# One change to a fused attention, mixer and routed-expert kernel: nine of twelve token tiles routed inside the last mixer block

## The chip, the cores and the metric

The kernel runs on one core of a Trainium2 chip. Its time is the device time of one execution in microseconds (us). Each engine of the core (TensorE, VectorE, ScalarE, GpSimd, SyncE) works through its own queue in order; semaphores tie the queues together. In rows, PE is TensorE's matmuls, PEld its weight loads, DVE is VectorE, ACT ScalarE, POOL GpSimd and SP SyncE.

## The reference

Three layers follow each other, all in fp32:

```python
def reference(...):
    attn_out = _attn_ref(q, k, v, n_global, n_local)      # (2, 8, 768, 64), windowed attention with bias
    x = attn_out.transpose(0, 2, 1, 3).reshape(B, S, H * D)   # (2, 768, 512)
    # mixer
    u = x + ((x.transpose(0, 2, 1) @ U) @ V).transpose(0, 2, 1)     # rank 32 over the sequence
    x = u + np.maximum(u @ w_ch1, 0) @ w_ch2                  # 512 -> 2048 -> 512
    # routed experts: E = 8, F = 1024
    logits = x @ w_gate;  local_gate = sigmoid(x @ w_local)
    for b in range(B):
        for s in range(S):
            fresh_e = argmax(logits[b, s])
            e = fresh_e if s == 0 or local_gate[b, s] < 0.5 else prev_e
            prev_e = e
            p = softmax(logits[b, s])
            out[b, s] = p[e] * (np.maximum(x[b, s] @ w1[e], 0) @ w2[e])
```

A token's expert depends on the token before it, where the local gate says so. The 1536 tokens are twelve token tiles of 128.

## The kernel before, in words

Every weight and activation is kept as a high and a low part (fp32r), and each product is three matmuls (`passes`, L477), so weights are cast on ScalarE (`split_hi`, L629) and their remainder made on VectorE (`split_lo`, L633), in eight units of 128 x 1024 for each of two weight buffers. `wbuf[0]` holds the mixer's first matrix, `wbuf[1]` its second; the experts then use the two by turns.

The mixer works in four blocks (kb) of three token tiles. A block has sixteen steps (f): `up` of f into a PSUM bank, `relu` on ScalarE (L714), its low part on VectorE (L751), and, one step behind, `down` of f-1 into three banks. At the end of a block VectorE adds the banks to `x` (`add_block`, L735), SyncE stores the three tiles to DRAM (`store_mixed`, L1205), and in steps 2 to 5 of the next block TensorE turns them and makes their gate logits (L544, L558), nine columns wide.

After the last block come the last three tiles' turning (L613) and logits (L620), and then, once logits of all twelve tiles are there, the routing: `route_dve` is a chain of small linked VectorE operations, each of which waits for the one before, and `route_pe_part` gives it TensorE's answers (turned rows L878, chain ends L882, carry L886, chain back L888, counts L891 to L893, places L898). The last of these is a 0/1 matmul that yields, for every expert tile, which token rows it takes and with which gate. GpSimd then gathers the 128 rows of the first expert tile from DRAM (`gather`, L1107, L1109), TensorE turns them (L932) and the loop over experts 0 to 7 begins. Each expert has one tile for every 128 of its tokens; while its first tile runs, the next expert's eight units are split. A tile is 24 `up` matmuls, 24 `down` matmuls and three groups of four transposes; its result is scaled (L1056) and scattered to the output (L1122) during the next tile.

TensorE's order around the change: all mixer steps, tail turns, tail logits, routing matmuls, first turn, tiles. ScalarE and VectorE split the first expert's units only after the mixer's last `up`, VectorE partly between routing operations. SyncE loads expert 0's first four units in the middle of the mixer, the other four in block 3.

## Time and profile before

| | |
|---|---|
| median of 3 runs | 631.56 us (631.07 to 634.59) |
| profiled execution, its own time | 633.74 us |
| its span, first to last instruction | 632.1 us |
| mean granted TensorE clock | 0.964 |
| TensorE busy | 590.1 us (93%), 3238 matmul instructions |
| VectorE / ScalarE / GpSimd busy | 267.6 / 242.9 / 125.5 us |
| last mixer block | 324.5 to 397.8 us of the span |
| first expert tile starts | 432.7 us |

An fp32 matmul shows as two instructions in a row's count, an fp32r one as one. Durations of neighbouring matmuls overlap, so the time from start to start is what a sequence takes. "[idle before <-releaser]" at the end of a row is how long the engine had sat idle and what ended it.

### The profile page before, as it was taken

To read this page: it belongs to the slowest core of one execution; us is meant where nothing else is said; L and a number is where in the kernel's file an instruction comes from. 1 tells how busy PE (TensorE), PEld (TensorE's weight loads), DVE (VectorE), ACT (ScalarE), POOL (GpSimd) and SP (SyncE) were. 2 spreads that over 40 slices of the span, in tenths; PEclk is the share of its full clock that TensorE was granted. 3 is DMA by queue.
4 is the path that set the end of the run, shared out by engine and by line. 5 is a ranking of instruction groups with operands and counts; after the bars stand their busy time and mean duration, and the time that the engine had idled before them with its cause. 6 is when DMAs were issued, how large, how long until landed. Compare 5 with 4: busy or idle time off the path is not lost.

```text
span 632.1 us, 9619 instructions
## 1 busy us (share of the span) xinstructions
PE 590.1 (93%) x3238; PEld 519.1 (82%) x3239; DVE 267.6 (42%) x566; ACT 242.9 (38%) x423; POOL 125.5 (20%) x160
## 2 busy tenths in 40 slices
PE   4999999999999999999999999646999999999995
PEld 4999898998899899999889999444787887888884
DVE  6565475444321221212221111785846278557311
ACT  6988584333112111111112011505734276537121
POOL 2999980000000000000000000002312122122121
PEclk9999997999999999999999999756999999999998
DMA  8678522433110000100000300535948169471110
GB/s 323 234 268 312 228 90 68 160 133 101 66 51 1 0 1 2 50 1 1 0 36 16 102 32 1 183 104 178 345 155 290 50 212 335 136 258 39 40 46 24
DMA packets 25252, 73.79 MB, mean 117 GB/s; under 512 B 2895, under 2 KB 4447, under 8 KB 25216
## 3 DMA queue, kind: packets, MB, share of 16 engines
q1 hardware_dynamic: 22128, 65.37, 29.1%
q0 software_dynamic: 2672, 7.62, 3.5%
q8 instruction: 21, 0.34, 0.2%
q10 hardware_dynamic: 416, 0.33, 0.2%
q14 instruction: 15, 0.12, 0.1%
HBM read 67.02 MB, written 7.34 MB: 118 GB/s over the span
## 4 chain that ended last, share of the span: by engine, by line
PE 76%; POOL 7%; DVE 6%; issue 5%; DMA 2%; ACT 2%; ACTq 1%; SPq 1%; DVEq 0%; POOLq 0%
PE bank L477 62%; POOL k_parts L1535 3%; DVE wbuf L633 3%; POOL q_parts L1532 2%; PE bank L959 2%; PE bank L521 2%; PE bank L1241 2%; DMA q_raw<-in_qT_dram 1%; PE bank L544 1%; POOL k_parts L1543 1%; PE bank L1253 1%; PE bank L1275 1%; PE bank L558 1%; PE bank L1274 1%; ACT wbuf L629 1%
## 5 line engine op out<-in xcount | busy, mean ns | idle before, releaser
L477 PE MATMUL bank<-uT,wbuf 128*128 128x384 f32 x768 | 149.4, 343 | 0.0
L477 PE MATMUL bank<-wbuf,hid 128*128 128x512 f32 x576 | 145.1, 396 | 0.0
L477 PEld LDWEIGHTS bank<-uT,wbuf 128*128 128x128 f32 x768 | 138.4, 191 | 7.8 <-issue 3.0
L751 DVE SCALAR_TENSOR_TENSOR hid<-bank,hid 128x384 fp32r<-128x384 f32 x64 | 35.7, 558 | 209.0 <-ACT hid L714 209.0
L477 PEld LDWEIGHTS bank<-wbuf,hid 128*128 128x128 f32 x576 | 106.0, 188 | 20.6 <-issue 0.8
L714 ACT ACTIVATE hid<-bank 128x384 fp32r<-128x384 f32 x64 | 31.4, 491 | 233.1 <-PE bank L477 233.1
L477 PE MATMUL bank<-wbuf,hT 128*128 128x512 f32 x360 | 89.7, 398 | 3.2 <-DVE hT L1066 3.1
L477 PE MATMUL bank<-wbuf,xT 128*128 128x512 f32 x360 | 90.2, 400 | 1.7 <-DVE xT L1048 1.7
L477 PEld LDWEIGHTS bank<-wbuf,xT 128*128 128x128 f32 x360 | 67.7, 192 | 15.7 <-issue 2.1
L477 PEld LDWEIGHTS bank<-wbuf,hT 128*128 128x128 f32 x360 | 65.3, 188 | 17.0 <-DVE wbuf L633 3.1
L1090 POOL IOTA rev<- 128x96 f32 x1 | 0.3, 293 | 300.4 <-PE bank L477 300.4
L1446 DVE CUSTOM_DVE_ANT_0 TS<-bank,bias 128x256 f32<-128x256 f32 (+1 forms) x96 | 34.6, 399 | 30.7 <-PE bank L1241 30.5
L1241 PE MATMUL bank<-k_parts,q_parts 128*128 128x256 f32 x192 | 38.0, 323 | 8.6 <-DVE k_parts L1428 7.3
L1340 ACT ACTIVATE PR<-TS,low 128x256 f32<-128x256 f32 (+1 forms) x96 | 41.9, 487 | 6.6 <-DVE low L1446 6.6
L1017 ACT ACTIVATE hs<-bank 128x512 f32<-128x512 f32 x30 | 17.9, 596 | 62.6 <-PE bank L477 62.6
L633 DVE TENSOR_TENSOR wbuf<-raw,wbuf 128x1024 fp32r<-128x1024 f32 x32 | 37.1, 1220 | 8.0 <-ACT wbuf L629 8.0
L1066 DVE TENSOR_TENSOR hT<-bank,hT 128x512 fp32r<-128x512 f32 x30 | 20.7, 690 | 44.5 <-ACT hT L1023 42.0
L1241 PEld LDWEIGHTS bank<-k_parts,q_parts 128*128 128x128 f32 x192 | 28.2, 201 | 12.1 <-DVE k_parts L1428 8.1
L633 DVE TENSOR_TENSOR wbuf<-late_raw,wbuf 128x1024 fp32r<-128x1024 f32 x32 | 37.6, 1216 | 0.0
L1122 POOL DMA_INDIRECT out_dram<-ys,give x16 | 18.1, 1131 | 85.2 <-DVE ys L1056 85.2
L629 ACT CAST wbuf<-raw 128x1024 fp32r<-128x1024 f32 x32 | 31.2, 1047 | 6.7 <-issue 6.7
L1535 POOL TENSOR_TENSOR k_parts<-k_raw,k_parts 128x640 fp32r<-128x640 f32 x21 | 32.6, 1552 | 1.7
(171 smaller groups left out, 640.4 us busy)
## 6 DMA issues: line engine op xcount, KB each, us to landing
raw<-in_w_dram SPq DMA_DIRECT2D x32, 512.0 KB, 4.8
late_raw<-in_w_dram SPq DMA_DIRECT2D x32, 512.0 KB, 4.6
raw<-in_w_ch_dram SPq DMA_DIRECT2D x16, 512.0 KB, 3.3
k_raw<-in_kT_dram SPq DMA_DIRECT2D x7, 960.0 KB, 4.9
vs<-in_vw_dram SPq DMA_DIRECT2D x8, 715.0 KB, 7.5
q_raw<-in_qT_dram SPq DMA_DIRECT2D x7, 768.0 KB, 6.5
mixed<-x SPq DMA_DIRECT2D x12, 256.0 KB, 2.1
q_raw<-in_qT_dram SPq DMA_DIRECT2D x3, 256.0 KB, 4.6
```

The lines of the kernel that those rows point to most:

```text
L477: last = pe.matmul(dst, lhs[a], rhs[b_], start=start and i == 0, stop=stop and i == 2)
L629: act.copy(w[:, 0, i, :], expert_slot(i)).then_inc(hi_split, 1)
L633: dve.tensor_tensor(w[:, 1, i, :], expert_slot(i), w[:, 0, i, :].bitcast(F32), ALU.subtract).then_inc(lo_split, 1)
L714: act.activation(hid[i % 2][:, 0, :], bank[3 + i % 2][:, 0:BN], ACT.Relu).then_inc(hid_hi, 1)
L751: dve.scalar_tensor_tensor(hid[i % 2][:, 1, :], bank[3 + i % 2][:, 0:BN], 0.0, hid[i % 2][:, 0, :].bitcast(F32), ALU.max, ALU.subtract).th ...
L1017: act.activation(hs[:, half, :], bank[3 + half][:, :], ACT.Relu).then_inc(e_relu, 1)
L1066: dve.tensor_tensor(hT[:, 1, half * NE // 2:(half + 1) * NE // 2, :], bank[5 + half][:, :].rearrange("p (c t) -> p c t", c=NE // 2), hT[:, ...
L1122: pool.indirect_dma_start(out=out_rows, out_offset=bass.IndirectOffsetOnAxis(ap=give[:, 0:1], axis=0), in_=ys[:, :], in_offset=None, bound ...
L1241: last = pe.matmul(score_bank[g % 2][:, h * WIN:(h + 1) * WIN], q_parts[:, par, h, t * P:(t + 1) * P], k_parts[:, par, a, h, start:start + ...
L1340: act.activation(PR[g % 3][:, h, 0:w], TS[g % 3][:, h, 0:w], ACT.Exp, bias=low[:, g, h:h + 1], scale=-1.0).then_inc(exped, 1)
L1446: dve.tensor_tensor_reduce(TS[g % 3][:, h, 0:w], score_bank[g % 2][:, h * WIN:h * WIN + w], bias[:, head % H, col], -SCALE, 3.0e38, ALU.ad ...
L1535: return pool.tensor_tensor(k_parts[:, par, 1, :, keys_of(c)], k_raw[par][:, :, keys_of(c)], k_parts[:, par, 0, :, keys_of(c)].bitcast(F32 ...
```

## The change

Only the order and the place of work change, and how slots are numbered.

1. The experts are no longer taken in order 0 to 7, but sorted by a count: in block 2, VectorE's `guess` marks the arg-max expert of each token in the first six tiles, a matmul with ones sums them (`guess_sum`), `sort` ranks the eight sums. SyncE waits for `order_ready` before it loads any expert weight.
2. In block 3 the first nine tiles are routed completely (`sure`, with TensorE's parts after `up` or `down` of steps 7 to 13). The first 128 tokens of each of the two first experts among these nine tiles are fixed as expert tiles 0 and 1. Tile 0's rows are gathered and turned at step 15.
3. The sixteen units of both first experts are split during block 3 into weight buffers as the mixer is through with each part (`FIRST_TWO_AT`), the last two during tile 0.
4. Expert tiles 0 and 1 follow the last `down` at once. Between their matmuls TensorE does the last three tiles' turning, logits, lines (the chain of the last 384 tokens on one partition), counts and the placing matmuls; VectorE does `late_head` to `late_index` between its shares of the two tiles. ScalarE waits for all mixed rows to be stored before the first `keep_h`.
5. The loop over experts starts with the rest of expert one, then the rest of expert two, then the other six. Slots in the tables grow from 21 to 25. The extra scaling and scatter of an empty tile at the start is gone.

The core of the diff:

```diff
+    SLOTS = NT + E + 5
+    REST = SLOTS - 2
+    STEPS = NT + 1
+    SURE = NT - BLK
+    GUESS = 2 * BLK
...
+                    if kb == NB - 2 and f == GUESS_SUM_AT:
+                        guess_sum(pe)
+                    if kb == NB - 1:
+                        sure_after_up(pe, f)
...
+        FIRST_TWO = [(0, 0), (0, 1), (1, 0), (0, 2), (1, 1), (0, 3), (1, 2), (0, 4),
+                     (1, 3), (0, 5), (0, 6), (1, 4), (1, 5), (0, 7), (1, 6), (1, 7)]
+        FIRST_TWO_AT = {2: (0,), 3: (1,), 4: (2,), 5: (3, 4), 7: (5,), 8: (6,), 9: (7,), 10: (8,),
+                        12: (9,), 13: (10,), 14: (11, 12), 15: (13,)}
+
+        def split_so_far(r, i):
+            return 2 * UNITS + FIRST_TWO.index((r, i)) + 1
+
+        def first_two_hi(act, k):
+            r, i = FIRST_TWO[k]
+            expert_raw(act, r, i)
+            last = (NB - 1) * NF + 2 * i + 2
+            act.wait_ge(*((up_done, last) if r == 0 else (down_step, last)))
...
+                        if f == EXP_AT:
+                            exponentiate(act, 0, SURE)
+                        for k in FIRST_TWO_AT.get(f, ()):
+                            first_two_hi(act, k)
+            act.sem_inc(e_relu, 2)
+            keep_x_hi(act, 0)
...
+                        if f == GUESS_SUM_AT - 2:
+                            router.guess()
+                        if f == GUESS_SUM_AT + 4:
+                            router.sort()
+                    if kb == NB - 1:
+                        router.sure(f)
+                        for k in FIRST_TWO_AT.get(f, ()):
...
+        def sure_after_up(pe, f):
+            if f == 9:
+                pe.wait_ge(route_go, 3)
+                for i in range(2):
+                    last = pe.matmul(bank[7][0:1, i * SURE:(i + 1) * SURE], chain[:, i, P - 1:P], ident[0:SURE, 0:SURE],
+                                     start=True, stop=True)
...
+            if f == 11:
+                pe.wait_ge(route_go, 6)
+                flat = "p e t -> p (e t)"
+                pe.matmul(bank[7][:, EARLY_COUNTS], before[:, :], OH[:, :, :].rearrange(flat), start=True, stop=False)
+                pe.matmul(bank[7][:, EARLY_COUNTS], ones[:, :], EXC[:, :, :].rearrange(flat), start=False, stop=True)
+                pe.matmul(bank[7][:, EARLY_SUMS], ones[:, :], CUM[:, :, SURE - 1], start=True, stop=True).then_inc(route_pe, 1)
+            if f == 13:
+                pe.wait_ge(route_go, 7)
+                for t in range(SURE):
+                    last = pe.matmul(bank[5][:, EARLY_PICKS], place[:, t, :],
+                                     sure_marks[:, t, :, :].rearrange("p i s -> p (i s)"), start=t == 0, stop=t == SURE - 1)
+                last.then_inc(route_pe, 1)
+            if f == NF - 1:
...
+        def late_lines(pe):
+            pe.wait_ge(route_go, 8)
+            for i, to in enumerate((bank[0][0:1, A_COLS], bank[1][0:1, B_COLS])):
+                for t in range(BLK):
+                    last = pe.matmul(to[:, t * P:(t + 1) * P], late_AB[:, i, t:t + 1], ident[:, :], start=True, stop=True)
             last.then_inc(route_pe, 1)
...
+        def late_picks(pe):
+            pe.wait_ge(route_go, 11)
             for t in range(NT):
-                if t % (NT // PLACE_PARTS) == 0:
-                    pe.wait_ge(place_ready, t // (NT // PLACE_PARTS) + 1)
-                last = pe.matmul(bank[4][:, 0:2 * SLOTS], place[:, t, :], marks[:, t, :, :].rearrange("p a g -> p (a g)"),
...
+            def guess(self):
+                dve, link = self.dve, self.link
+                dve.wait_ge(late_ready, 9)
+                link(dve.tensor_reduce(top[:, 0:GUESS], LG[:, 0:GUESS, 0:E], AX, ALU.max))
+                link(dve.tensor_tensor(eq0[:, :, :], LG[:, 0:GUESS, 0:E], inner(top[:, 0:GUESS], GUESS, E), ALU.is_ge))
+                self.hand(dve.tensor_reduce(per[:, 0, :], eq0[:, :, :].rearrange("p t e -> p e t"), AX, ALU.add))
...
+            def sort(self):
+                dve, link = self.dve, self.link
+                dve.wait_ge(route_pe, 1)
+                link(dve.scalar_tensor_tensor(per[:, 1, :], bank[7][:, EARLY_SUMS], float(E), rev[:, :], ALU.mult, ALU.add))
+                link(dve.tensor_tensor(above[:, :, :], outer(per[:, 1, :], E, E), inner(per[:, 1, :], E, E), ALU.is_gt))
+                link(dve.tensor_reduce(per[:, 2, :], above[:, :, :], AX, ALU.add))
+                link(dve.tensor_tensor(sel[:, :, :], outer(per[:, 2, :], E, E), inner(which[:, :], E, E), ALU.is_equal))
+                link(dve.tensor_tensor(pairs_e[:, :, :], sel[:, :, :], outer(which[:, :], E, E), ALU.mult))
+                link(dve.tensor_reduce(per[:, 3, :], pairs_e[:, :, :], AX, ALU.add))
+                link(dve.tensor_tensor(per[:, 4, :], sel[:, 0, :], sel[:, 1, :], ALU.add))
+                dve.tensor_copy(order[:, :], per[0:1, 3, :]).then_inc(order_ready, 1)
...
+            def sure(self, f):
+                dve, link, hand = self.dve, self.link, self.hand
+                part = slice(0, SURE)
+                if f == 6:
+                    dve.wait_ge(late_ready, 12)
+                    self.head(0, SURE, AB)
+                    hand(dve.tensor_tensor(AB[:, 1, :], cols[:, 1, part], cols[:, 0, part], ALU.mult))
...
+                if f == 9:
+                    dve.wait_ge(route_pe, 3)
+                    link(dve.tensor_copy(ends[:, :, :], bank[7][0:1, 0:2 * SURE].rearrange("o (a t) -> o a t", a=2)))
+                    hand(dve.tensor_tensor_scan(carry[:, 1:SURE + 1], ends[:, 1, :], ends[:, 0, :], 0.0, ALU.mult, ALU.add))
+                    dve.wait_ge(route_pe, 4)
+                    link(dve.tensor_copy(carried[:, :], bank[7][0:SURE, 32:33]))
+                    hand(dve.scalar_tensor_tensor(chain[:, 0, :], chain[:, 1, :], carried[:, 0:1], chain[:, 0, :],
+                                                  ALU.mult, ALU.add))
+                if f == 10:
+                    flat = "p e t -> p (e t)"
+                    dve.wait_ge(route_pe, 5)
+                    link(dve.tensor_copy(cols[:, 2, part], bank[5][:, EARLY_BACK]))
...
+                    hand(dve.tensor_tensor(EXC[:, :, :], CUM[:, :, :], OH[:, :, :], ALU.subtract))
+                    self.gates(0, SURE)
+                if f == 11:
+                    dve.wait_ge(route_pe, 6)
+
+                    link(dve.tensor_copy(per[:, 5, :], bank[7][:, EARLY_SUMS]))
+                    link(dve.scalar_tensor_tensor(per[:, 5, :], per[:, 4, :], float(P), per[:, 5, :], ALU.mult, ALU.max))
+                    link(dve.tensor_tensor(CUM[:, :, :], bank[7][:, EARLY_COUNTS].rearrange("p (e t) -> p e t", e=E),
...
+                    link(dve.tensor_scalar(cols[:, 9, part], cols[:, 7, part], 0.5, None, ALU.is_lt))
+                    link(dve.tensor_tensor(fixed[:, :, :], fixed[:, :, :], outer(cols[:, 9, part], 2, SURE), ALU.mult))
+                if f == 12:
+                    link(dve.tensor_tensor(cols[:, 9, part], fixed[:, 0, :], fixed[:, 1, :], ALU.add))
+                    link(dve.scalar_tensor_tensor(cols[:, 7, part], cols[:, 9, part], MASKED, cols[:, 7, part], ALU.mult, ALU.add))
+                    for i, value in enumerate((left[:, part], cols[:, 6, part])):
+                        link(dve.tensor_tensor(sure_marks[:, :, i, :], fixed[:, :, :].rearrange("p s t -> p t s"),
+                                               inner(value, SURE, 2), ALU.mult))
+                    hand(self.put(0, SURE))
+                if f == 13:
+                    dve.wait_ge(route_pe, 7)
+                    index = IX[:, 1:3, 0]
+                    link(dve.tensor_scalar(index, bank[5][:, 300:302], -1.0, float(T), ALU.mult, ALU.add))
+                    dve.tensor_scalar(GI[:, 0:2], index, float(SURE * P - 1), None, ALU.min).then_inc(gi_ready, 1)
+                    link(dve.tensor_copy(IX[:, 1:3, 1].bitcast(F32), bank[5][:, 302:304]))
+
...
+            def late_marks(self):
+                dve, link = self.dve, self.link
+                part = slice(SURE, NT)
+                dve.wait_ge(route_pe, 10)
+                link(dve.tensor_tensor(per[:, 6, :], bank[0][:, SUMS], per[:, 5, :], ALU.add))
...
+                link(dve.tensor_reduce(cols[:, 9, :], eq[:, :, :], AX, ALU.add))
+                link(dve.tensor_tensor(cols[:, 9, :], cols[:, 9, :], cols[:, 7, :], ALU.add))
+                link(dve.tensor_tensor(hit[:, :, :], inner(cols[:, 9, :], NT, REST), outer(rest_cols[:, :], NT, REST), ALU.is_equal))
+                for i, value in enumerate((left[:, :], cols[:, 6, :])):
+                    link(dve.tensor_tensor(marks[:, :, i, :], hit[:, :, :], inner(value, NT, REST), ALU.mult))
+                self.hand(self.put(SURE, BLK))
+
+            def tables(self):
...
+            own = own_first(0)
+            pe.wait_ge(xT_lo, 1)
+            up(0, 0, 0, range(DC // 2), own)
+            tail_turns(pe)
+            up(0, 0, 0, range(DC // 2, DC), own)
+            tail_logits(pe)
+            up(0, 0, 1, range(DC // 2), none)
+            turn_h(0, 0)
+            up(0, 0, 1, range(DC // 2, DC), none)
+            late_lines(pe)
+            turn_x(pe, 1)
+            down(0, 0, range(1), own)
+            turn_h(0, 1)
+            late_back(pe)
+            down(0, 0, range(1, 3), own)
+            late_counts(pe)
+            down(0, 0, range(3, NE), own)
+
+            own = own_first(1)
+            pe.wait_ge(xT_lo, 2)
+            up(1, 1, 0, range(DC), own)
+            up(1, 1, 1, range(DC // 2), none)
+            turn_h(1, 0)
+            up(1, 1, 1, range(DC // 2, DC), none)
+            late_picks(pe)
+            down(1, 1, range(1), own)
+            turn_h(1, 1)
+            down(1, 1, range(1, 5), own)
+            turn_x(pe, 2)
+            down(1, 1, range(5, NE), own)
+
+            def own_unit(r, i):
+                wait_loop(pe, lo_split, UNITS * (r + 2) + i + 1)
 
             def tile(g, par, unit, own):
...
+            relu(0, 0)
+            first_two_hi(act, 14)
+            exponentiate(act, SURE, BLK)
+            act.wait_ge(u2_out, 16 * NT)
+            keep_h(0, 0)
+            first_two_hi(act, 15)
+            relu(0, 1)
+            keep_x_hi(act, 1)
+            keep_h(0, 1)
+            relu(1, 0)
+            keep_h(1, 0)
+            relu(1, 1)
+            keep_h(1, 1)
+            keep_x_hi(act, 2)
...
+            router.late_head()
+            first_two_lo(dve, 14)
+            keep_h(0, 0)
+            first_two_lo(dve, 15)
+            router.late_line()
+            keep_x_lo(dve, 1)
+            router.late_ranks()
+            keep_h(0, 1)
+            router.gates(SURE, BLK)
+            router.late_marks()
+            scale_y(1)
+            router.tables()
+            keep_h(1, 0)
+            router.late_index()
+            keep_h(1, 1)
+            keep_x_lo(dve, 2)
+
...
+            for j in range(NT - 2 * BLK):
+                store_mixed(j)
+            sp.wait_ge(order_ready, 1)
+            e_of = [sp.value_load(order[0:1, r:r + 1], min_val=0, max_val=E - 1) for r in range(2)]
             for i in range(RAW):
                 sp.wait_ge(lo_split, 2 * UNITS - RAW + i + 1)
-                load_expert_unit(0, i)
-            for j in range(NT - BLK):
+                load_expert_unit(0, e_of[0], i)
+            for j in range(NT - 2 * BLK, NT - BLK):
                 store_mixed(j)
...
+            def load_second(i):
+                sp.wait_ge(lo_split, split_so_far(0, i))
+                load_expert_unit(1, e_of[1], i)
```

## Rows read from the trace of the kernel before

**Rows 1.** The page's 40 slices of 15.8 us: busy tenths, and granted clock.

```profile
PE   4999999999999999999999999646999999999995
PEclk9999997999999999999999999756999999999998
```

**Rows 2.** Table by stage: stretch, length, busy of PE, PEld, DVE, ACT, POOL, then clock, DMA.

```profile
324.46:397.77 73.31, 73.31 (x382) 66.05 (x380) 13.26 (x22) 13.17 (x23) 1.56 (x12) 1.00 0.11 40
397.77:402.60 4.83, 4.05 (x35) 3.69 (x34) 4.15 (x5) 1.95 (x4) 0.00 (x0) 0.99 0.68 232
402.60:432.68 30.08, 10.71 (x50) 9.03 (x50) 18.47 (x57) 5.19 (x8) 1.97 (x4) 0.50 0.41 137
...
461.58:473.85 12.27, 12.27 (x62) 10.19 (x60) 4.37 (x6) 5.47 (x8) 2.38 (x4) 1.00 0.34 108
...
436.00:436.50 0.50, 0.50 (x3) 0.40 (x2) 0.50 (x2) 0.50 (x2) 0.00 (x0) 0.50 0.89 246
```

**Rows 3.** The page's costliest groups: busy, mean ns, idle before.

```profile
L751 DVE SCALAR_TENSOR_TENSOR hid<-bank,hid 128x384 fp32r<-128x384 f32 x64 | 35.7, 558 | 209.0 <-ACT hid L714 209.0
...
L477 PE MATMUL bank<-wbuf,hT 128*128 128x512 f32 x360 | 89.7, 398 | 3.2 <-DVE hT L1066 3.1
...
L633 DVE TENSOR_TENSOR wbuf<-raw,wbuf 128x1024 fp32r<-128x1024 f32 x32 | 37.1, 1220 | 8.0 <-ACT wbuf L629 8.0
...
L629 ACT CAST wbuf<-raw 128x1024 fp32r<-128x1024 f32 x32 | 31.2, 1047 | 6.7 <-issue 6.7
```

**Rows 4.** Timeline of TensorE over the expert tiles: start, length, line.

```profile
432.68 6.23 PE L477 MATMUL bank<-wbuf,xT 128*128 128x512 f32 x18 [1.67 <-DVE xT L1048]
...
448.17 4.25 PE L477 MATMUL bank<-wbuf,xT 128*128 128x512 f32 x18
452.26 0.60 PE L959 MATMUL bank<-ident,hs 128*128 128x128 f32 x4
452.61 1.63 PE L477 MATMUL bank<-wbuf,xT 128*128 128x512 f32 x6
...
611.84 4.25 PE L477 MATMUL bank<-wbuf,xT 128*128 128x512 f32 x18
```

**Rows 5.** Timeline of all engines in the routing chain, at a granted clock of 0.50.

```profile
404.23 0.26 DVE L791 SCALAR_TENSOR_TENSOR eq<-shl,rev 128x96 f32<-128x96 f32 x1
...
405.66 1.03 PE L878 MATMUL bank<-ident,AB 128*12 128x128 f32 x4 [2.33 <-DVE AB L797]
...
406.79 0.41 DVE L806 COPY rows<-bank 12x256 f32<-12x256 f32 x1 [0.43 <-PE bank L878]
407.24 0.41 DVE L807 TENSOR_TENSOR_SCAN chain<-rows 12x128 f32<-12x128 f32 x1
...
411.72 0.74 PE L891 MATMUL bank<-OH,before 128*128 128x96 f32 x2 [1.31 <-DVE EXC L824]
...
418.47 1.89 DVE L857 TENSOR_TENSOR place<-places,cols 128x512 f32<-128x512 f32 x3
419.21 5.35 PE L898 MATMUL bank<-marks,place 128*128 128x42 f32 x24 [6.04 <-DVE place L857]
```

**Rows 6.** Timeline around the first gather.

```profile
424.87 0.18 DVE L870 TENSOR_SCALAR GI<-IX 128x21 int32<-128x21 int32 x1
...
429.90 1.12 PE L932 MATMUL bank<-ident,xs 128*128 128x128 f32 x4 [5.34 <-DMA xs<-mixed,take]
```

**Rows 7.** Timeline of TensorE in block 3: two logit rows, two step starts.

```profile
340.19 0.96 PE L558 MATMUL bank<-gate_sb,u2T 128*128 128x9 f32 x8
...
341.00 2.29 PE L477 MATMUL bank<-wbuf,hid 128*128 128x512 f32 x9
...
374.64 2.27 PE L477 MATMUL bank<-uT,wbuf 128*128 128x384 f32 x12
...
378.82 2.27 PE L477 MATMUL bank<-uT,wbuf 128*128 128x384 f32 x12
```

**Rows 8.** The page's DMA issues: KB each, median us to landing.

```profile
raw<-in_w_dram SPq DMA_DIRECT2D x32, 512.0 KB, 4.8
...
mixed<-x SPq DMA_DIRECT2D x12, 256.0 KB, 2.1
```

More of the change, by code:

```diff
@@ L109, in build @@
+        IX = sb("IX", [P, SLOTS + NT + 4, 2], I32, over_h)
+        GI = sb("GI", [P, SLOTS + NT + 4], I32, over_h)
+        take = sb("take", [P, 1], I32, over_h)
+        give = sb("give", [P, 1], I32, over_h)
+        ends = sb("ends", [1, 2, SURE], F32, over_h)
+        carry = sb("carry", [1, SURE + 1], F32, over_h)
+        carried = sb("carried", [SURE, 1], F32, over_h)
+        over_h.close()
+        sb("mixing_room", [P, TB * 3 * R + S + B * DM], F32)
         early = ExitStack()
@@ L277, in build @@
         route = sem("route")
+        route_go = sem("route_go")
+        shl_ready = sem("shl_ready")
+        order_ready = sem("order_ready")
         route_pe = sem("route_pe")
@@ new lines, in sure_after_down @@
+        def sure_after_down(pe, f):
+            if f == 7:
+                pe.wait_ge(route_go, 2)
+                for i in range(2):
+                    last = pe.matmul(bank[5][0:SURE, i * P:(i + 1) * P], AB[:, i, :], ident[:, :], start=True, stop=True)
+                last.then_inc(route_pe, 1)
+            if f == 9:
+                pe.wait_ge(route_go, 4)
+                pe.matmul(bank[7][0:SURE, 32:33], carry[:, 0:SURE], ones[0:1, 0:1], start=True, stop=True).then_inc(route_pe, 1)
@@ L879, in route_pe_part, with late_back @@
+        def late_lines(pe):
[3 more added lines that the diff above has]
+                    last = pe.matmul(to[:, t * P:(t + 1) * P], late_AB[:, i, t:t + 1], ident[:, :], start=True, stop=True)
             last.then_inc(route_pe, 1)
-            pe.wait_ge(route, 14)
-            for i in range(2):
-                last = pe.matmul(bank[1][0:1, i * NT:(i + 1) * NT], chain[:, i, P - 1:P], ident[0:NT, 0:NT],
+        def late_back(pe):
+            pe.wait_ge(route_go, 9)
+            for t in range(BLK):
+                last = pe.matmul(bank[0][:, BACK + t:BACK + t + 1], line[:, 1, t * P:(t + 1) * P], ones[0:1, 0:1],
@@ L922, in last_expert, with turn_x, x_bank @@
+            base = eng.value_load(table[0:1, 2 * E - 1:2 * E], min_val=3, max_val=SLOTS)
             return tiles, base
+        def turn_x(pe, g):
+            to = bank[6] if isinstance(g, int) and g == 0 else bank[2]
+            wait_loop(pe, xs_in, 16 * (g + 1))
+            for c in range(DC):
+                last = pe.transpose(to[:, c * P:(c + 1) * P], xs[:, c * P:(c + 1) * P], ident[:, :])
+            last.then_inc(xT_done, 1)
+        def x_bank(g):
+            return (bank[6] if isinstance(g, int) and g == 0 else bank[2])[:, :].rearrange("p (c t) -> p c t", c=DC)
@@ L976, in tile @@
-                for c in range(DC):
-                    own(c)
-                    up(0, range(c, c + 1))
-                up(1, range(DC // 2))
-                turn_h(0)
-                up(1, range(DC // 2, DC))
-                turn_x(g + 1)
-                down(range(1))
-                turn_h(1)
-                down(range(1, NE))
+                up(g, par, 0, range(DC), own)
+                up(g, par, 1, range(DC // 2), none)
+                turn_h(g, 0)
+                up(g, par, 1, range(DC // 2, DC), none)
@@ L987, in experts_pe @@
+                turn_x(pe, g + 1)
+                down(g, par, range(1), own)
+                turn_h(g, 1)
+                down(g, par, range(1, NE), own)
             experts(pe, tile, own_unit=own_unit)
```

661 lines of the change are left out of this document (367 added, 294 removed).

## The prediction, made before the result was known

> **What bounds the kernel now.** I read the slices of the page first [rows 1]: TensorE is busy in nearly all of them except slices 27 to 29 (6, 4 and 6 tenths), and there its clock falls as well. So the kernel is bound by TensorE everywhere but in one place. The table by stage then puts bounds on that place [rows 2]: the last mixer block (324.46 to 397.77) is 100% busy; 397.77 to 402.60 is transposes and gate logits; 402.60 to 432.68 has 10.7 us of TensorE work in 30.1 us, at a granted 0.50, which is the 1.2 GHz level; from 432.68 come fifteen expert tiles (360 matmuls of hT [rows 3] at 24 each). The timeline of TensorE gives their starts, first and last of fifteen in [rows 4]. The steps are 15.49, 13.41, 12.27, 12.88, 12.27, 12.28, 12.60, 13.42, 12.26, 12.62, 12.27, 12.82, 12.27, 12.30, and 12.3 for the last. An undisturbed tile is 12.27, as that from 461.58 to 473.85 [rows 2]. The first pays 3.22 more (its first 3.8 us run at 1.2 GHz: still a granted 0.50 in 436.0 to 436.5 [rows 2]), and the first tile of most experts 0.3 to 1.15 more, for the split of the next expert's weights.
>
> Last mixer matmul to third expert tile is 461.58 - 397.77 = 63.8 us, of which two tiles at 12.27 are 24.5. The other 39.3 us are what the change can touch: a chain of routing steps in which each engine waits for the other [rows 5], then the gather [rows 6].
>
> **What is taken away.** The whole 63.8 us stretch, to be replaced as follows. The work for nine token tiles goes into mixer block 3 (and the count of six into block 2), and tiles 0 and 1 run with the routing of the last three token tiles between their matmuls.
>
> **Put into the last block, on TensorE.** At half clock the trace has 1.03 for the 4 instructions that turn AB, 0.26 each, and 0.74 for the first 2 of the 6 that count [rows 5]; at 2.4 GHz that is 0.5, and 0.9 for the counts, which follow each other more closely. The chain's ends, the carry and the way back are 8 narrower instructions, at most 0.13 each: I take 0.5, between 0.2 and 1.0. So 1.9 us. The placing matmuls take 5.35 for 24 at half clock, 0.22 each, so 0.11 each at full (the gate logits, also fp32 and narrow, take 0.81 for 8, 0.10 each: the row starts at 340.19 and the next at 341.00, [rows 7]). Nine token tiles are 18 instructions: 2.0. The sum over experts 0.2, turning tile 0's rows 0.36 (four transposes: the next matmul starts 0.35 after them, 452.26 to 452.61, [rows 4]). Together 4.5 us.
>
> **Put into the last block, on VectorE and ScalarE.** One step of the block is 4.19 us (374.64 to 378.82 [rows 7]), in which VectorE works 0.56 [rows 3] and ScalarE 0.5. Fourteen unit splits are added at 1.22 and 1.05 [rows 3]. Routing operations of 96 elements cost 0.26, shorter ones 0.2, and 0.41 go to the copy of the rows and to a scan [rows 5], and linked ones follow at 0.03 more. Per step f, hid, splits and routing for VectorE: f5 0.56 + 2.44, f6 0.56 + 0.2 + 2.0, f8 0.56 + 1.35 + 1.22, f9 0.56 + 1.1 + 0.7 waiting for TensorE's carry + 1.22, f10 0.56 + 1.1 + 1.9 + 1.22 = 4.8, f11 0.56 + 3.5, f12 0.56 + 0.8 + 1.35 (the put over 9 x 128 by 0.63 for 4 x 128, [rows 5]) + 1.22. All fit in 4.19 but f10, by 0.6, and hid of f has the time of down(f-1) and up(f+1) before down(f) asks for it. So no hid is late. For the early TensorE steps: it asks for route_go 3, 5, 6, 7 after up 9, 10, 11, 13; by the sums the values are there 1 to 2.5 us before. The first gather starts 2.5 us after up(13); gather rows show 4.85 us from GI to TensorE's turn [rows 6], while three down/up pairs and the picks give it 8. Hidden. The units: slots free in the order of the splits, 512 KB land in 4.8 [rows 8], each is asked for at least one step of 4.19 later and mostly two. SyncE now waits for order_ready before any expert load; sort gives it at step f13 of block 2, five steps (over 20 us) before the first split of a unit, and only stores stand behind it. I charge 0.5 us for VectorE lateness in this block; the bounds are 0 and, if every one of the seven handoffs were 1 us late, 7.
>
> **In the two tiles.** On TensorE: 2 x 12.27 = 24.5. Tail transposes 3 x 0.35 = 1.1. Logits 3 x 0.81 = 2.4. late_lines is three column turns of two kinds, 12 instructions at half of 1.03/4: 1.5. late_back 0.4, late_counts 0.9, late_picks 24 x 0.11 = 2.6. Sum 33.4. Stalls, with T = 0 at the start of tile 0: the logits end at 11.1 (u2_done is there: add_block's three at 0.63 run under the first six matmuls). VectorE's late_head is nine operations, done at 13.5; TensorE reaches late_lines at 14.3. Behind it on VectorE stand split 14, keep_h, split 15 (1.22 + 0.69 + 1.22), so late_line starts at 16.6, and its copy and scan of 384 elements on one partition take about 0.55 + 0.8 (from 0.41 for 256 copied and for 128 scanned [rows 5]): 18.1. TensorE waits for it from 17.0: stall 1.1. late_counts: 0.2 at most. late_ranks, gates and late_marks are about 33 small operations, some 9 us, done near 28; late_picks is reached at 29.8. No stall. ScalarE's new wait for all twelve stores (u2_out) has keep_h(0, 0), split 15 and relu(0, 1) behind it; stores go out by T + 3 and land in 2.1 [rows 8], and keep_h could not start before turn_h at 8 us more. Then late_picks to turn_x(2): the same path takes 5.3 now (idle of TensorE before the turn, [rows 6]); between stand four transposes, five chunks and a turn, 3.8 us. Stall 1.5. Together 33.4 + 2.8 = 36.2. I add 1.0 for about a dozen more changes of kind on TensorE, none of which the trace prices in this order (0 to 2).
>
> **Behind them.** From the reference with its drawn inputs I count 117, 192, 308, 104, 181, 226, 230, 178 tokens per expert: 15 tiles by 128, as in the trace. First nine tiles hold 225 for expert 2 and 161 for expert 4, which the count of six puts first (163, 122), so both fixed tiles are full: still 15, order 2, 4, 6, 1, 3, 5, 7, 0. Excess over 12.27 in the last thirteen is 3.1 now. After: five first-tile splits behind an expert of several tiles (0.6 x 4 and 0.33 for the single tile), one behind the single-tile expert (1.15): 3.9. So +0.8, and +0.5 for entering the loop in the middle (at the borders between experts TensorE shows no gap now).
>
> Sum: 63.8 - 36.2 - 1.0 - 4.5 - 0.5 - 0.8 - 0.5 = 20.3 us gained. The profiled execution took 633.74 (span 632.1 and 1.6 around it): 613.4 there. It lies 2.2 above the median of the runs, so 611.3 on that scale; I say **611**.
>
> **A rule beside it.** The clock fell at 402.60 after 4.8 us in which TensorE was 84% busy with transposes and nine-column logits [rows 2], and came back 3.8 us into dense work. The Trainium skill, "TensorE: Matmul & The Clock Gate", section "What's actually happening", says the default state is throttled and activity releases it, by how busy the engine has been. This trace agrees on the return and not on the fall, before which the engine hardly rested. By the rule the new tiles, in which TensorE hardly rests, hold 2.4 GHz and the sum stays; by the row they may lose it, and that is the second rival.
>
> **Rivals.**
> - *Handoffs late inside the block.* ScalarE or VectorE falls a step behind, because splits and routing share in-order queues: the split of unit k waits for its load or for ScalarE, and the routing operation behind it makes TensorE wait. For: f10 is already over its step, and SyncE's loads stand one behind the other. Against: at 0.56 of 4.19 busy there is much air. Price: 3 to 8 us more, 614 to 619.
> - *The clock dips once.* In tile 0 tail turns, six matmuls, logits, six matmuls, then lines and a stall follow each other; in f13 the placing. A busy TensorE loses half of each us at 1.2 GHz; low for 10 to 15 us, as long as the new tile 0, it loses 5 to 7.5: 616 to 618.5. Against: no run of small matmuls is over 2.6 us there, and block 3 of now, with logits of 0.81 in three of its steps, stays at 1.00 [rows 2].
> - *Slower.* The clock falls in block 3 at the first handoff that waits (f9) and isn't given back, because the waits come every step until turn_x(2). Matmuls at 1.2 GHz take twice the time; it decides once over 20 us of full-clock work runs so. From f9 to turn_x(2) are some 65 us of work; half of it at 1.2 GHz gives 611 + 32 = 643. For: the clock of now stayed low from 402.6 to past 436 [rows 2]. Against: 3.8 us of dense matmuls ended it, and block steps are dense.
> - *The late part isn't hidden* (the change doesn't do what it says): gi_ready 2 comes late because VectorE's queue with about 50 small operations is the chain, and turn_x(2) waits 8 rather than 1.5: 617. For: 0.29 for each link is all latency. Against: 12 us of tile 1 lie before the picks need it.
>
> **Chances.** Forecast with its own range 606 to 614: 0.60. Late handoffs 0.15, clock dip once 0.08, late part 0.09, slower 0.05; 0.03 for less than 606. Low end: no stalls (2.8), no changes of kind (1.0), no lateness (0.5), no excess (1.3): 605.7; I give 604.5. High end 620 takes in the rivals that still gain. A measurement of this kernel tells 0.5%, 3 us, from no change: faster 0.93, same 0.02, slower 0.05.
>
> **What would show it.** TensorE's idle inside 324 to 400 at most 1 us and VectorE near 44 us busy there; the block longer by 4 to 5.5 us; PEclk 1.00 until the last tile; tile 0 begins within 0.3 us of the last down matmul; between that and the third tile 35 to 39 us; waits of TensorE on line and on xs of 1 to 2 us each; fifteen tiles. A PEclk under 1.00 before the end, a wait over 2 us on place, chain or hid, or sixteen tiles would make the forecast wrong.

## The result and the profile after

The changed kernel takes 610.59 us (median of 4 runs, 609.97 to 613.6), beside 631.73 us for the kernel before on the same chip: a ratio of 0.9664, with a 95% interval of 0.9645 to 0.9684. That is 21.1 us less; 20.3 us had been forecast. Its profiled execution took 610.67 us, with a span of 608.8, against 633.74 and 632.1.

The page's slices answer to [rows 1]:

```profile
PE   4999999999999999999999999999999999999994
...
PEclk9999998999999999999999999999999999999998
```

The hole of slices 27 to 29 is gone, and so is the low clock in it. By stages, with the same columns as [rows 2]: the first row is the last mixer block from its third step on, the second is tiles 0 and 1 with the late routing, then come tile 2, which is undisturbed, and the first tile of the third expert.

```profile
331.85:401.46 69.61, 69.61 (x380) 62.35 (x379) 36.41 (x77) 22.38 (x33) 3.69 (x5) 1.00 0.27 88
401.46:437.38 35.92, 34.83 (x206) 29.20 (x205) 20.79 (x64) 9.48 (x16) 3.23 (x5) 1.00 0.48 175
437.38:449.67 12.29, 12.29 (x62) 10.19 (x60) 2.83 (x4) 2.85 (x5) 2.76 (x6) 1.00 0.21 64
...
474.25:487.59 13.34, 12.57 (x62) 10.22 (x60) 10.70 (x12) 7.66 (x11) 3.63 (x4) 1.00 0.95 343
```

The same steps of the last block, before:

```profile
333.03:397.60 64.57, 64.57 (x340) 58.51 (x338) 10.26 (x17) 12.01 (x21) 1.56 (x12) 1.00 0.10 33
```

The timeline of TensorE through tiles 0 and 1 of the changed kernel (start, length, line, what; idle before it in brackets):

```profile
401.46 1.53 PE L506 MATMUL bank<-wbuf,xT 128*128 128x512 f32 x6
402.83 1.48 PE L647 MATMUL bank<-ident,x 128*128 128x128 f32 x12
404.06 1.64 PE L506 MATMUL bank<-wbuf,xT 128*128 128x512 f32 x6
405.53 2.74 PE L655 MATMUL bank<-gate_sb,tail_u2T 128*128 128x9 f32 x24
...
411.51 1.47 PE L882 MATMUL bank<-ident,late_AB 128*1 128x128 f32 x12
412.92 0.66 PE L1162 MATMUL bank<-ident,xs 128*128 128x128 f32 x4
...
415.00 0.82 PE L888 MATMUL bank<-ones,line 1*128 1x1 f32 x6 [0.30 <-DVE line L1063]
...
421.35 4.25 PE L506 MATMUL bank<-wbuf,xT 128*128 128x512 f32 x18
...
427.26 2.77 PE L902 MATMUL bank<-marks,place 128*128 128x46 f32 x24
...
434.80 0.66 PE L1162 MATMUL bank<-ident,xs 128*128 128x128 f32 x4 [0.79 <-DMA xs<-mixed,take]
```

Between the last down matmul and the first of tile 0 nothing is idle. In the whole stretch TensorE waits twice, 0.30 us for the line and 0.79 us for the third tile's rows. The placing matmuls that took 5.35 us in [rows 5] take 2.77.

From the starts, the span's 23.3 us divide so:

| stretch | before | after | difference |
|---|---|---|---|
| start to third step of block 3 | 333.03 | 331.85 | -1.2 |
| from there to the end of the mixer (397.60, 401.46) | 64.6 | 69.6 | +5.0 |
| end of the mixer to tile 2 | 64.0 | 35.9 | -28.1 |
| tile 2 to the end of tile 14 | 162.6 | 163.4 | +0.85 |
| end | 8.0 | 8.0 | 0 |

The first line is no work of the change. Nearly all of it is there early in the mixer: the `up` that starts at 112.63 us before starts at 111.34 after. It lies in the attention phase, where this stretch of the two kernels, first before and then after, shows a different mean clock for the same code:

```profile
90.00:110.00 20.00, 18.86 (x126) 18.34 (x126) 12.69 (x38) 11.57 (x22) 3.03 (x2) 0.83 0.17 56
```

```profile
90.00:110.00 20.00, 18.86 (x135) 18.21 (x135) 13.70 (x41) 12.17 (x24) 3.26 (x2) 0.91 0.17 56
```

The second profile of the changed kernel, below, has 0.83 there too, and seven of its variants have 1.00 (in the version with doubled splits the same `up` starts at 110.52). So spans of single executions differ by 1 to 2 us for that alone, and medians are what I compare.

### The profile page after: what moved, and what is told of

It reads as the page before. It is cut to its first block, busy times and chain, and to the rows that moved or that the text cites. A ratio compares the mean times of both kernels' runs of the same rounds, so it can differ in the third digit from the quotient of the medians.

```text
span 608.8 us, 9641 instructions
## 1 busy us (share of the span) xinstructions
PE 587.0 (96%) x3282; PEld 516.9 (85%) x3283; DVE 279.0 (46%) x623; ACT 242.6 (40%) x423; POOL 125.2 (21%) x160
## 4 chain that ended last, share of the span: by engine, by line
PE 80%; POOL 7%; DVE 4%; issue 3%; DMA 2%; ACT 1%; SPq 1%; DVEq 1%; ACTq 0%; POOLq 0%
PE bank L506 65%; POOL k_parts L1857 3%; POOL q_parts L1854 2%; DVE wbuf L668 2%; PE bank L550 2%; PE bank L1195 2%; PE bank L1562 2%; DMA q_raw<-in_qT_dram 2%; PE bank L573 2%; POOL k_parts L1865 1%; PE bank L1574 1%; PE bank L1596 1%; PE bank L587 1%; PE bank L1595 1%; PE bank L1162 1%
## 5 line engine op out<-in xcount | busy, mean ns | idle before, releaser
L506 PE MATMUL bank<-wbuf,xT 128*128 128x512 f32 x360 | 88.8, 394 | 0.0
L506 PEld LDWEIGHTS bank<-wbuf,hT 128*128 128x128 f32 x360 | 65.2, 188 | 15.8 <-DVE wbuf L668 2.0
L506 PEld LDWEIGHTS bank<-wbuf,xT 128*128 128x128 f32 x360 | 66.3, 188 | 13.1
L664 ACT CAST wbuf<-late_raw 128x1024 fp32r<-128x1024 f32 x32 | 32.8, 1046 | 0.0
```

The lines of the kernel that those rows point to most:

```text
L506: last = pe.matmul(dst, lhs[a], rhs[b_], start=start and i == 0, stop=stop and i == 2)
L664: act.copy(w[:, 0, i, :], expert_slot(i)).then_inc(hi_split, 1)
```

## The experiments

All were timed against the kernel before on the same chip; ratios have their 95% intervals. The medians of the kernel before in these groups are 631.7 to 632.5 us, and the changed kernel's two medians are 610.59 and 611.62, so between groups a difference of about 1 us says nothing.

**The sort taken out.** In `sort`:

```diff
-                link(dve.scalar_tensor_tensor(per[:, 1, :], bank[7][:, EARLY_SUMS], float(E), rev[:, :], ALU.mult, ALU.add))
+                link(dve.scalar_tensor_tensor(per[:, 1, :], bank[7][:, EARLY_SUMS], 0.0, rev[:, :], ALU.mult, ALU.add))
```

> The changed kernel with the experts in order 0 to 7 (the count is multiplied by 0 before ranking), all else equal. Theory: the sort is worth one expert tile. Experts 0 and 1 hold only 82 and 123 of the first nine tiles' tokens, their first tile is then closed, and expert 0's 117 tokens need a second one: sixteen tiles (384 matmuls of hT instead of 360), 12.3 us more, 622 to 624 us. Rival: the order does not matter, the slots come out alike, 610 to 612 us and 360 matmuls.

Measured: 623.4 us, ratio 0.9861 (0.9841 to 0.9881), 12.8 us over the changed kernel. The timeline has fifteen starts of an `up` of 18 after tile 0 rather than fourteen, and the page has 384 matmuls of hT:

```profile
L506 PE MATMUL bank<-wbuf,hT 128*128 128x512 f32 x384 | 96.5, 399 | 2.7 <-DVE hT L1331 2.5
```

A tile that is closed before all tokens are known costs nothing if it is full, or if what comes later needs no more tiles than before. With expert 0 first the tile holds 82 rows, and the 35 that come later need a tile of their own. Expert 1's tile, closed with 123 rows, costs nothing, because its 192 tokens take two tiles either way. The sort secures 12.8 of the 21.1 us.

**The late part in one piece.** TensorE runs tail turns, logits, lines, back, counts and picks, and only then tile 0; VectorE and ScalarE follow in that order:

```diff
-            up(0, 0, 0, range(DC // 2), own)
             tail_turns(pe)
-            up(0, 0, 0, range(DC // 2, DC), own)
             tail_logits(pe)
+            late_lines(pe)
+            late_back(pe)
+            late_counts(pe)
+            late_picks(pe)
+            up(0, 0, 0, range(DC), own)
...
-            late_picks(pe)
```

> The changed kernel with the last three tiles' routing (turns, logits, lines, counts, placing) in one piece ahead of expert tile 0 instead of between the matmuls of tiles 0 and 1. Theory: what tiles 0 and 1 hide is VectorE's and the handoffs' time: some 27 us of chain of which 8.8 are TensorE's either way, so 16 to 18 us come back, and 2 to 4 more if the clock falls to 1.2 GHz in the gap: 626 to 632 us. Rival (the gain came from routing nine tiles early, and the late part is short by itself): at most 8 us more, 612 to 619 us.

Measured: 628.27 us, ratio 0.9936 (0.9919 to 0.9953): 17.7 us come back. The chain ahead of tile 0 and the two tiles, by stage:

```profile
400.90:427.80 26.90, 15.09 (x85) 13.19 (x85) 12.26 (x46) 1.88 (x4) 0.00 (x0) 0.60 0.45 170
427.80:455.50 27.70, 27.63 (x122) 22.31 (x123) 8.71 (x18) 7.58 (x12) 3.26 (x5) 0.90 0.18 57
```

54.6 us instead of 35.9, at a granted clock of 0.60 and 0.90. Its biggest wait is again that for the last placing:

```profile
422.65 5.35 PE L902 MATMUL bank<-marks,place 128*128 128x46 f32 x24 [5.97 <-DVE place L992]
```

From the mixer's last matmul to the end of the placing it is 26.9 us (400.88 to 427.79), and 26.8 in the kernel before (397.77 to 424.56), although only three tiles are left to route instead of twelve. So all of the rest (nine tiles routed early, units split early, the sort) is worth 3.7 us by itself, and laying the last three tiles' routing under two expert tiles that are known by then is worth 17.7, nearly five times that. The rival is out. This 17.7 and the sort's 12.8 are not parts of one sum: together they are more than the 21.1 us, as each experiment takes one piece out of the finished whole.

**The clock held in the kernel before.** Dense matmuls on data that nothing reads, in TensorE's waits:

```diff
+        def fill(pe, n):
+            for _ in range(n):
+                pe.matmul(bank[5][:, :], wbuf[1][:, 0, 6, 0:P], wbuf[1][:, 0, 6, 0:DM], start=True, stop=True)
+
         def route_pe_part(pe):
+            fill(pe, 10)
             pe.wait_ge(route, 8)
...
+            fill(pe, 22)
             turn_x(0)
+            fill(pe, 6)
```

> The kernel before, with 79 dense matmuls of 128 x 512 put into the waits of TensorE between tail logits and first expert tile (their result is read by nothing). Theory: holding 2.4 GHz is worth the half-rate part only, 3 us of routing matmuls and 2 of tile 0, less some collision of fillers with the chain: 625 to 630 us, clock 1.00 in the gap. Rival: the clock is most of the 21 us: under 618 us.

Measured: 631.15 us, ratio 0.999 (0.9974 to 1.0006). The forecast of 2 to 7 us less was wrong. The placing matmuls are at full clock, and VectorE is not there to read them:

```profile
417.41 2.87 PE L908 MATMUL bank<-marks,place 128*128 128x42 f32 x24 [0.64 <-DVE place L857]
...
418.62 3.48 DVE L633 TENSOR_TENSOR wbuf<-late_raw,wbuf 128x1024 fp32r<-128x1024 f32 x3
...
422.28 0.18 DVE L869 TENSOR_SCALAR IX<-bank 128x21 int32<-128x21 f32 x1
```

They end at 420.28; VectorE is in three splits until 422.05. In the kernel before, at half clock, the same three had ended under the matmuls, which went on to 424.56:

```profile
420.42 3.48 DVE L633 TENSOR_TENSOR wbuf<-late_raw,wbuf 128x1024 fp32r<-128x1024 f32 x3
```

The added matmuls also have a price of their own here: tile 0's rows are ready at 429.94, and tile 0 starts at 430.88, behind the last six of them, at a granted 0.50 from 428.3 on. To test the first reading, the same with those splits behind the index copies:

```diff
-            first_expert_lo(dve, 5, UNITS)
...
             link(dve.tensor_copy(IX[:, 1:SLOTS + 1, 1].bitcast(F32), bank[4][:, SLOTS:2 * SLOTS]))
+            first_expert_lo(dve, 5, UNITS)
```

> The kernel before with the same 79 dense matmuls in TensorE's waits, and VectorE's last three splits of the first expert behind the index copies instead of ahead of them. Theory: with the clock held, the placing matmuls end 2 us before VectorE is through with those splits, which is where the gain of the dense matmuls went; now it shows, 1.5 to 3.5 us less than before: 628 to 630 us. Rival: the fillers cost what the clock gives, 631 to 632 us as with them alone.

Measured: 630.35 us, ratio 0.9972 (0.9956 to 0.9988), short of the forecast's 630 by 0.35: a gain of 1.9 us (0.8 to 2.8 by the interval), inside the forecast gain of 1.5 to 3.5. The gap is 2.5 us shorter, at a granted 1.00, but tile 0 is no faster for its full clock:

```profile
396.96:429.30 32.34, 29.20 (x162) 22.67 (x161) 22.75 (x62) 7.12 (x11) 1.95 (x4) 1.00 0.47 162
429.32:444.89 15.57, 12.90 (x60) 10.23 (x61) 12.85 (x13) 13.20 (x17) 5.13 (x6) 1.00 0.75 254
```

It takes 15.57 us against 15.49 before. TensorE waits 2.0 us in it for ScalarE's relu, which stands behind six splits that start with the tile:

```profile
429.36 3.90 ACT L629 CAST wbuf<-raw 128x1024 fp32r<-128x1024 f32 x4 [1.02 <-issue]
433.16 1.99 ACT L629 CAST wbuf<-late_raw 128x1024 fp32r<-128x1024 f32 x2
435.05 0.59 ACT L1028 ACTIVATE hs<-bank 128x512 f32<-128x512 f32 x1
...
435.69 0.66 PE L970 MATMUL bank<-ident,hs 128*128 128x128 f32 x4 [1.99 <-ACT hs L1028]
```

The low clock of slices 27 to 29 was mostly a companion of the gap: holding it gives back about 2 of the 21 us. It may be a little more, as the first gather landed 1.3 us later in this version than before (last section), and no run separates that.

**VectorE loaded in the last block.** Each of the fourteen low-part splits done twice:

```diff
             dve.wait_ge(hi_split, split_so_far(r, i))
+            if k < 14:
+                dve.tensor_tensor(wbuf[r][:, 1, i, :], expert_slot(i), wbuf[r][:, 0, i, :].bitcast(F32), ALU.subtract).then_inc(twice, 1)
+                dve.wait_ge(twice, k + 1)
             split_lo(dve, wbuf[r], i)
```

> The changed kernel with each of the fourteen low-part splits of the last mixer block done twice on VectorE (1.22 us more in each, 17 us in all). Theory: a low part of hid may be about 3 us late and the routing values come 1 to 2 us before they are asked for, so most of it is absorbed: 1 to 4 us more, 611.5 to 615 us. Rival (VectorE is at its limit in the block and every split shows): 8 to 17 us more, 619 to 628 us.

Measured: 613.13 us, ratio 0.9702 (0.9685 to 0.972), 2.5 us over the changed kernel's first runs and 1.5 over its second, inside the forecast. The block from its third step goes from 69.6 to 70.9 us, with VectorE busy 52.9 us in 71.9. Of 17 us put in, 1.3 show there, and where they show is the end of the block:

```profile
398.97 2.35 PE L507 MATMUL bank<-wbuf,hid 128*128 128x512 f32 x9 [0.18 <-DVE hid L807]
401.96 1.66 PE L507 MATMUL bank<-wbuf,xT 128*128 128x512 f32 x6 [0.64 <-DVE xT L1178]
```

None of the routing handoffs makes TensorE wait. The rival of late handoffs is far off.

**The late part delayed.** Forty small linked operations in front of the last placing:

```diff
+                for _ in range(40):
+                    link(dve.tensor_tensor(top[:, part], cols[:, 8, part], cols[:, 8, part], ALU.mult))
                 self.hand(self.put(SURE, BLK))
```

> The changed kernel with 40 small linked operations (0.2 us each, 8 us) on VectorE in late_marks, ahead of the last placing: nothing uses their result. Theory: the trace has placing done at 424.6 and asked for at 427.2, 2.6 us of room, so 5 to 6.5 us come through: 615.5 to 617.5 us. Rival (the late part is hidden with room to spare, as 12 us of tile 1 suggest): less than 2 us more.

Measured: 619.86 us, ratio 0.9813 (0.9791 to 0.9834), 9.3 us over the changed kernel's first runs and 8.2 over its second, and 2.4 above the forecast's upper end. The 7.8 us of delay give a wait of 5.06, so the room of 2.6 us is right:

```profile
424.53 7.80 DVE L1102 TENSOR_TENSOR top<-cols 128x3 f32<-128x3 f32 x40
...
432.98 5.35 PE L902 MATMUL bank<-marks,place 128*128 128x46 f32 x24 [5.06 <-DVE place L992]
```

What was left out of the forecast is what follows the wait: the matmuls behind it run at a granted 0.50 and then 0.79,

```profile
432.98:440.00 7.02, 7.02 (x30) 6.62 (x31) 2.86 (x11) 0.00 (x0) 1.39 (x3) 0.50 0.11 40
440.00:446.78 6.78, 6.78 (x28) 5.59 (x27) 1.38 (x2) 1.18 (x2) 1.81 (x3) 0.79 0.12 39
```

and the 10.1 us from the placing to tile 2 become 13.8. In these tiles, where TensorE is the bound, the 5.1 us wait costs 8.8.

**The remaining waits.** The changed kernel once more, and two versions of it. In the loop over tiles, on VectorE:

```diff
                 unit(DC)
+                keep_h(g, 0)
                 unit(DC + 1)
-                keep_h(g, 0)
                 keep_x_lo(dve, g + 1)
```

and, in the second version, also in tiles 0 and 1:

```diff
-            first_two_lo(dve, 15)
             router.late_line()
             keep_x_lo(dve, 1)
             router.late_ranks()
             keep_h(0, 1)
+            first_two_lo(dve, 15)
...
-            down(1, 1, range(1, 5), own)
+            down(1, 1, range(1, 6), own)
             turn_x(pe, 2)
-            down(1, 1, range(5, NE), own)
+            down(1, 1, range(6, NE), own)
```

> The changed kernel itself, beside the next two on the same chip. Both theories: 610 to 611.5 us.

> The changed kernel with one swap on VectorE in the loop over tiles: the low part of hT's first half ahead of the split of unit 5 instead of behind it. Theory: the 0.3 to 1.07 us that the first tile of an expert takes over 12.28 is TensorE's wait for that low part behind two splits, 2.3 us in all; the swap takes most of it: 608 to 609.5 us. Rival: the splits are only moved, and the tile waits for the next expert's units instead: 610 to 612 us.

> The same swap, and in tiles 0 and 1 split 15 behind late_ranks and keep_h(0, 1) instead of ahead of late_line, and the turn of tile 2's rows one down chunk later. Theory: the waits of TensorE for line (0.30) and for the gathered rows (0.79) go as well, 1.1 us less than with the swap alone: 607 to 608.5 us. Rival: they turn up at the next handoff, same as the swap alone.

Measured: 611.62 us (0.9678, 0.9661 to 0.9696), 607.9 us (0.9613, 0.9591 to 0.9636) and 606.64 us (0.9603, 0.9588 to 0.9618). The first lies 0.1 above its forecast, the two others 0.1 and 0.4 below theirs. The swap gives 3.7 us: from tile 2's start to tile 14's, 147.6 us instead of 151.1, each step 12.28 to 12.32. The third expert's first tile, before the swap and with it:

```profile
478.35 2.35 DVE L668 TENSOR_TENSOR wbuf<-late_raw,wbuf 128x1024 fp32r<-128x1024 f32 x2
480.61 0.68 DVE L1331 TENSOR_TENSOR hT<-bank,hT 128x512 fp32r<-128x512 f32 x1
...
481.54 0.96 PE L506 MATMUL bank<-wbuf,hT 128*128 128x512 f32 x3 [0.77 <-DVE hT L1331]
```

```profile
481.73 1.21 DVE L668 TENSOR_TENSOR wbuf<-late_raw,wbuf 128x1024 fp32r<-128x1024 f32 x1
482.97 0.69 DVE L1331 TENSOR_TENSOR hT<-bank,hT 128x512 fp32r<-128x512 f32 x1
...
483.91 0.96 PE L506 MATMUL bank<-wbuf,hT 128*128 128x512 f32 x3
```

The 0.3 to 1.07 us of an expert's first tile were all that one low part behind two splits. With the other two moves the waits for the line and for the rows go from 0.30 and 0.79 to none and 0.17:

```profile
433.93 0.66 PE L1162 MATMUL bank<-ident,xs 128*128 128x128 f32 x4 [0.17 <-DMA xs<-mixed,take]
```

By the trace that takes 0.7 us from tiles 0 and 1 together (35.2 instead of 35.9); the medians with and without the two moves lie 1.3 us apart, and their intervals overlap. This last version beats both kernels, by 4% and by 0.8%.

**The low stretch in tile 0.** The second profile of the changed kernel has what its first has not, 3.4 us at 1.2 GHz near 410:

```profile
408.00:412.00 4.00, 4.00 (x24) 3.69 (x25) 1.24 (x7) 1.43 (x3) 0.00 (x0) 0.74 0.95 310
412.00:414.00 2.00, 2.00 (x9) 1.57 (x8) 1.76 (x4) 0.18 (x1) 0.00 (x0) 0.67 0.97 377
```

It makes tile 0 take 21.1 us instead of 19.9. The versions without the sort, with the swap alone and with the delayed late part have it too; the others do not (the version with the late part in one piece has no such tile 0). I tried to tell whether the tail turns and logits, nearly in a row there, bring it: one version with each tile's logits between three `up` matmuls (and with VectorE's split 15 moved behind `keep_h(0, 1)`), one with turns and logits directly in a row, and one with the logits apart and all moves of the last paragraph.

```diff
-            tail_logits(pe)
-            up(0, 0, 1, range(DC // 2), none)
+            tail_logits(pe, range(1))
+            up(0, 0, 1, range(1), none)
+            tail_logits(pe, range(1, 2))
+            up(0, 0, 1, range(1, 2), none)
+            tail_logits(pe, range(2, 3))
+            up(0, 0, 1, range(2, 3), none)
...
```

```diff
             up(0, 0, 0, range(DC // 2), own)
+            up(0, 0, 0, range(DC // 2, DC), own)
             tail_turns(pe)
-            up(0, 0, 0, range(DC // 2, DC), own)
             tail_logits(pe)
```

> The changed kernel with the last three tiles' logits apart, one tile's at a time between the up matmuls of tile 0, and lines, back and counts one or two chunks later. Theory: the 3.4 us at 1.2 GHz that some executions of the changed kernel have near 408 to 410 comes of turns and logits nearly in a row; apart, no execution has it: mean clocks of 0.994 and more except where the attention phase has its own low stretch, and 610 to 611 us. Rival: the low stretch has nothing to do with the logits and is there as often as before.

> The changed kernel with tail turns and tail logits directly behind each other, without the six matmuls between. Theory: the low stretch near 408 is then there in every execution, and TensorE waits some 0.7 us for the first copy: 2 to 3.5 us more, 612.5 to 615 us. Rival: the order does not touch the clock, only the wait shows: 611 to 612 us.

> The logits spread, with the swap in the loop and the later turn of tile 2's rows. Theory: as the version with swap and later turn, less the executions with the low stretch: 606 to 607 us, nothing over 608. Rival: the later lines push the last placing past what tile 1 hides, 608 to 610 us.

Measured: 610.33 us (0.9677, 0.9651 to 0.9703), 611.13 us (0.967, 0.9651 to 0.9689) and 606.84 us (0.9601, 0.9581 to 0.9621). The forecast for turns and logits in a row fell: the profiled execution stays at 1.00 right through, and all five have a mean clock of 0.994 or more:

```profile
404.00:408.00 4.00, 4.00 (x36) 3.77 (x34) 0.00 (x0) 2.96 (x5) 0.00 (x0) 1.00 1.00 343
408.00:412.00 4.00, 4.00 (x24) 3.11 (x24) 2.97 (x12) 1.71 (x5) 0.00 (x0) 1.00 0.94 353
```

The forecast for the logits apart is not decided. Two of its five runs are near 613 us at a mean clock of 0.992, but it had excepted executions with a low stretch in the attention phase, and these two were not profiled. Their 2.3 to 2.8 us more are nearer to what that stretch costs (2.1 us between a granted 0.83 and 1.00, from the starts at 112.63 and 110.52 above) than to tile 0's 1.2. The third version came out as forecast, nothing over 608. So what brings the low stretch of tile 0 in some executions stays open; what it costs, 1.2 us, does not.

## Why the prediction was right

- *What bounds the kernel.* Right: TensorE everywhere but in one gap. The 39.3 us beyond two tiles became 11.4.
- *The sum, and some luck in it.* Added up in the forecast's own terms, the traces give 64.0 - 35.9 - 5.0 - 0.85 = 22.2 us instead of 20.3: 1.3 from the two tiles, 0.45 from what lies behind them, 0.2 from the stretch taken away. The medians lie 21.1 apart, so the number came out closer (0.4 us, or 0.07%, from the forecast 611) than the terms. The profiled execution before lay 2.0 us above its median and the one after lay at its median. The clock of the attention phase can be 1.2 of that; the rest is not accounted for.
- *Into the last block, on TensorE, 4.5 us and 0.5 for lateness.* Measured 5.0. From start to start the groups take 4.0: nine tiles' picks 1.9, counts 0.6 (0.9 foreseen), AB 0.5, the rest near the forecast. The other 1.0 is spread over the changes between wide and narrow matmuls and is not VectorE's lateness, for which the text had 0.5: in front of these groups TensorE waits for nothing. So in this term errors of 0.5, 1.0 and 0.5 cancel. VectorE is busy 39.0 us between 324 and 400, not near 44.
- *In the two tiles, 33.4 us of work, 2.8 of stalls, 1.0 for changes of kind.* Measured 35.9: 34.8 of work with its changes of kind, 1.1 of stalls. The two stalls came at the places and for the reasons given, but smaller. One slip of the text: its T is the end of the last `up`, 4.8 us before tile 0 starts, not that start. From there (396.7) VectorE was to have the line at 18.1 and has it at 18.3; TensorE was to ask at 17.0 and, for the changes of kind, asks at 18.0. For the rows, the path took 4.9 rather than 5.3 us and what lies beside it 4.2 rather than 3.8.
- *Behind them, +0.8 and +0.5.* Measured +0.85; entering the loop in the middle costs nothing. The rest of the 1.3 was too much. The parts: 1.07 rather than 0.6 in the third expert's first tile, and nothing in the second expert's last.
- *The rivals.* Late handoffs: excluded, by the block without a wait and by the doubled splits. A late last part: its room is 2.6 us, where the text had 1.8. The clock dipping once: it is real, in four of ten profiled executions of the changed kernel and its variants (the late part in one piece left out), but lasts 3.4 us and costs 1.2, not 5 to 7.5. A clock under 1.00 before the end was named as a sign that would make the forecast wrong; it was too strict a sign. Its lasting through the block was not seen. Where TensorE is made to wait 5 us, in the version with the delayed late part, the clock stays low for 10.2 us.
- *What the text had wrong about the kernel before.* It explained the first tile's 3.22 us by 3.8 us at 1.2 GHz, which by its own rule of half of each us are 1.9. With the clock held and the splits behind the index copies the tile takes 15.57: ScalarE's splits bound it just as late. The sum did not suffer, as the whole 3.22 was taken as gone.
- *The rule beside it.* The return of the clock in dense work agrees with "What's actually happening" of the Trainium skill's page "TensorE: Matmul & The Clock Gate" in every run here. For the fall without rest the runs have rows on both sides: [rows 2], where TensorE was 84% busy, and 408 to 414 of the second profile, where it was busy throughout, against the turns and logits in a row, which kept 1.00.

## What to carry to other kernels

A serial chain of small handoffs need not get shorter when most of its data is dealt with earlier (26.9 us for three tiles, 26.8 for twelve); it goes when work whose inputs are already certain is laid over what is left. Choosing that work so that it costs no extra tile (here by sorting on a partial count) was worth 12.8 us. Where one queue holds both bulk work and the one operation that the bound engine waits for, put that operation ahead of the last bulk item: one swapped pair of lines gave 3.5 us between the starts of tiles 2 and 14. A low clock next to a gap is no proof of a cost; hold it, and see what the gap still waits for.

## What the runs showed of the hardware that was not expected

The granted clock of one and the same code differs between executions: 0.83, 0.91 or 1.00 in the stretch of 90 to 110 us, and 1.00 or 0.74 at 408 to 412, which spreads the times of one kernel by 1 to 3 us. A row of 22 dense matmuls did not keep it either where 2.45 us of waiting followed: in the first version with added matmuls the clock was low for 3.4 us from 428.3, at the start of tile 0. In the second, where the wait was 1.51 us, it stayed at 1.00. After the 5.06 us wait of the delayed version TensorE was busy with the narrow placing matmuls from 432.98 to 438.12, at 0.50 throughout; the clock rose near 442.8, in the dense matmuls behind them. The first gather landed later in the version with splits behind the index copies: 6.3 us from index to turn, against 5.0 before [rows 6]. Three 512 KB loads were issued there from 422.30 on, beside the gather at 422.08, and before they had been issued from 421.66 on, ahead of the gather at 426.20. That these loads are the cause is not shown, since the DMA engines are 0.90 and 0.98 busy in 425 to 428 before as well.
